# New orders in the opening of a linear-attention and expert kernel: lanes in three buffers, another bank for the first w, half of X loaded from ScalarE's queue

## The chip, the cores and the metric

The kernel runs on one core of one Trainium2 chip. The metric is the device time in microseconds (us), the median of the runs. The core has TensorE (PE), VectorE (DVE), ScalarE (ACT), GpSimd (POOL) and SyncE (SP), whose queue here only issues DMAs. Each engine works through its own instructions in the order written and waits on semaphores.

## What is computed

A recurrent attention over 768 tokens for 4 batches of 8 heads of size 40, then a gated expert layer and a second one over the 3072 x 320 result:

```python
for t in range(S):
    y[:, :, t] = np.einsum('bhd,bhde->bhe', rt, state)
    Sa = np.einsum('bhde,bhe->bhd', state, at)
    state_decay = state * wt[:, :, None, :] - np.einsum('bhd,bhe->bhde', Sa, bt)
    state = state_decay + np.einsum('bhd,bhe->bhde', vt, kt)
...
h = (x @ w1) * (x @ w2) @ w3
x = h @ w_out
out = np.maximum(x @ w_in, 0.0) ** 2 @ w_out2
```

## The kernel before

The recurrence is cut into 24 windows (n): 64 tokens of two of the four batches, all heads in pairs side by side. Even and odd windows are the two halves of the batches, so window n takes its state from window n - 2. For each window TensorE turns w, a and r (ar), b and k (bk) with transposes (`turn_w`, `turn_ar`, `turn_bk`); VectorE forms the running product of w (`scan`), its reciprocal (`invert_decay`, two parts), and scales a and bk by them (`scale_a`, `scale_bk`). `cross` multiplies them to 64 x 64 blocks in PSUM; `mask_ak` on VectorE copies the odd half's 32-row diagonal blocks to `diag` and masks the products; `copy_blocks` on ScalarE copies the even half's blocks to `diag` and the off-diagonal ones to `n10`. `fill_lanes` on VectorE transposes `diag` into the tile `blk` (two slots, n % 2), and GpSimd's `invert` solves the triangular blocks with 62 dependent small operations after a seed copy: windows 0 and 1 each alone, 2 and 3 in one joint pass, and each later one alone. It waits first for `inverse_turned` (the earlier inverse has left `inv`), then for `lanes_filled`. `turn_inverse` on VectorE turns the result to `invT`. Then comes the window's dependent chain: `make_z`, `make_u0`, `make_x1`, `add_x1`, `make_u1`, `turn_uv`, `add_state`, `new_state`, `make_read`, `mask_read`, `make_y`, `turn_state`, `scale_y`, with copies out of PSUM on ScalarE between them (`copy_x`, `copy_u`, `copy_uvT`, `copy_state`). Windows 0 and 2 use the PSUM tensor `both` and 1 and 3 `aside`; from 4 on all use `both`, since the experts take `aside`.

y goes to DRAM (`store_y`, tensor xT) and comes back as X (`load_x`, x_raw), is split into a rounded and a rest part (`round_x` on ScalarE, `rest_x` on VectorE) and multiplied with split weights. The products of w3 and w_out are folded once in the opening: `turn_w3(ft)` and four `multiply_w3(ft, part)` for each of 8 row blocks, then `round_fold`, `rest_of_fold`, `store_fold`. The weights come by `load_staged`, w_out as `load_wo`.

The opening is the first four windows and the fold; its order is written out by hand, one list for each engine. After it a loop over windows 4 to 23 weaves the window's steps with steps of the expert layers (`next(beside)`), and after window 23 only experts are left. The first expert matmul (xT_hi, `into_hidden`) stands in that loop after the whole opening list of TensorE. The lists wait across engines: on SyncE `next_w(n)`, `next_ar(n)` and `next_bk(n)` wait for the transposes of window n - 1, since each raw tile has one buffer; `load_x` waits until the stores of y have landed; `store_fold(ft)` waits for `rest_of_fold(ft)`.

## Time and profile before

| | us |
|---|---|
| median of 3 runs (lowest, highest) | 1009.25 (1007.94, 1013.59) |
| the profiled execution | 1012.14 |
| its span | 1010.4 |
| busy in the span: PE, DVE, POOL, ACT | 953.6, 653.9, 448.4, 424.6 |
| first expert matmul | 138.49 |

The profile is one execution. Busy time is the time in which an engine's instructions run; matmuls are pipelined and their ends modelled. A line of a timeline gives start, duration, engine, line of the kernel, operation, output and input tiles, the count of merged instructions, and in brackets the idle time of the engine in front and what ended it. PEclk is the granted TensorE clock as a share of 2.4 GHz. DMA share is the mean busy share of the 16 DMA engines.

### The profile page before, as it was taken

The page shows a single profiled execution, that of the slowest core. Times are in us where ns is not written, and L with a number is a line of the kernel's source. Part 1 is how long each engine was busy: PE and PEld are TensorE (multiplying, and loading weights), DVE is VectorE, ACT ScalarE, POOL GpSimd, SP SyncE. Part 2 cuts the span into 40 slices and gives each one's busy share as a digit, 9 for nine tenths or more (in the row PEclk, how much of TensorE's full clock was granted, in tenths as well). Part 3 has the DMA queues.
Part 4 walks back from the last instruction along what each step waited for, and adds up shares of the span by engine and source line. Part 5 has one row for each costly group of instructions (what it writes and reads, how often), then busy time and mean ns, then how long its engine had stood idle before and what let it go on. Part 6 is the DMA issues. An engine that isn't in the chain of part 4 may idle for free.

```text
span 1010.4 us, 34808 instructions
## 1 busy us (share of the span) xinstructions
PE 953.6 (94%) x14560; PEld 775.6 (77%) x14560; DVE 653.9 (65%) x1101; ACT 424.6 (42%) x904; POOL 448.4 (44%) x1464
## 2 busy tenths in 40 slices
PE   5877898989898999999999999999999999999998
PEld 4665666778787778887778887778887778888797
DVE  7877556788866567667577677577677575442433
ACT  3443444455544344444345444344344344432332
POOL 2778725537446265365355355355356355100000
PEclk8999789999989999999999999999999999999999
DMA  9965466757868757658756759765758743565552
GB/s 178 180 148 124 106 153 182 187 164 229 235 203 235 148 145 168 160 145 229 168 143 161 176 140 228 158 149 154 178 146 221 158 130 123 178 205 180 156 159 78
DMA packets 267804, 169.52 MB, mean 168 GB/s; under 512 B 200064, under 2 KB 229760, under 8 KB 267648
## 3 DMA queue, kind: packets, MB, share of 16 engines
q1 hardware_dynamic: 267648, 167.29, 64.8%
q8 instruction: 116, 1.90, 0.8%
q14 instruction: 40, 0.33, 0.1%
HBM read 141.03 MB, written 26.21 MB: 166 GB/s over the span
## 4 chain that ended last, share of the span: by engine, by line
PE 69%; DVE 4%; POOL 2%; issue 2%; ACT 1%; DVEq 0%
PE aside L908 29%; PE moe_bank L995 16%; PE moe_bank L980 8%; PE both L871 2%; PE both L763 2%; PE both L886 2%; PE both L804 1%; PE both L795 1%; PE both L857 1%; PE both L776 1%; POOL inv L703 1%; PE both L882 1%; POOL inv_tmp L700 1%; PE both L743 1%; DVE h_lo L1588 1%
## 5 line engine op out<-in xcount | busy, mean ns | idle before, releaser
L700 POOL TENSOR_TENSOR inv_tmp<-blk,inv 128x60 f32<-128x60 f32 (+26 forms) x713 | 205.7, 288 | 356.2 <-DVE blk L1511 302.0
L703 POOL TENSOR_TENSOR inv<-inv,inv_tmp 128x60 f32<-128x60 f32 (+26 forms) x713 | 230.9, 324 | 55.8
L995 PE MATMUL moe_bank<-v_ring,h_hi 128*128 128x320 f32 x768 | 177.1, 318 | 0.0
L908 PE MATMUL aside<-xT_hi,w_ring 128*128 128x512 f32 x480 | 150.3, 411 | 3.5 <-DVE h_lo L1588 3.5
L908 PE MATMUL aside<-x2T_hi,w_ring 128*128 128x512 f32 x480 | 148.5, 407 | 4.0 <-DVE h_lo L1588 3.9
L995 PEld LDWEIGHTS moe_bank<-v_ring,h_hi 128*128 128x128 f32 x768 | 128.7, 189 | 6.1
L1588 DVE TENSOR_TENSOR h_lo<-aside,h_hi 128x512 fp32r<-128x512 f32 x144 | 97.4, 676 | 49.2 <-ACT h_hi L1290 49.1
L1598 DVE SCALAR_TENSOR_TENSOR aside<-aside,left 128x512 f32<-128x512 f32 x96 | 66.7, 695 | 95.3 <-ACT left L1298 95.1
L1290 ACT CAST h_hi<-aside 128x512 fp32r<-128x512 f32 x144 | 84.6, 588 | 95.6 <-DVE aside L1598 52.5
L995 PE MATMUL moe_bank<-v_ring,h_lo 128*128 128x320 f32 x384 | 119.2, 310 | 0.0
L1298 ACT ACTIVATE left<-aside 128x512 f32<-128x512 f32 x96 | 57.5, 598 | 115.9 <-PE aside L908 115.7
L908 PEld LDWEIGHTS aside<-xT_hi,w_ring 128*128 128x128 f32 x480 | 85.4, 189 | 22.0 <-DVE h_lo L1588 5.0
L908 PEld LDWEIGHTS aside<-x2T_hi,w_ring 128*128 128x128 f32 x480 | 84.1, 188 | 22.0 <-issue 5.4
L908 PE MATMUL aside<-xT_lo,w_ring 128*128 128x512 f32 x288 | 98.2, 395 | 0.0
L908 PE MATMUL aside<-x2T_lo,w_ring 128*128 128x512 f32 x288 | 97.0, 391 | 0.0
L1475 DVE RECIPROCAL undecay<-decay 104x256 f32<-104x256 f32 x48 | 83.4, 1740 | 0.2
L980 PE MATMUL moe_bank<-h_hi,v_ring 128*128 128x512 f32 x240 | 81.6, 405 | 0.0
L1236 ACT COPY uv<-both 32x160 f32<-32x160 f32 x176 | 49.8, 283 | 61.4 <-PE both L804 59.8
L995 PEld LDWEIGHTS moe_bank<-v_ring,h_lo 128*128 128x128 f32 x384 | 72.7, 189 | 0.0
L1596 DVE TENSOR_TENSOR aside<-left,aside 128x512 f32<-128x512 f32 x48 | 33.0, 687 | 55.0 <-PE aside L908 54.7
L908 PEld LDWEIGHTS aside<-xT_lo,w_ring 128*128 128x128 f32 x288 | 54.9, 191 | 12.5
L908 PEld LDWEIGHTS aside<-x2T_lo,w_ring 128*128 128x128 f32 x288 | 54.1, 188 | 12.5 <-DVE x2T_lo L1630 0.2
...
## 6 DMA issues: line engine op xcount, KB each, us to landing
...
```

The costliest lines, as they stand in the source:

```text
L700: nc.gpsimd.tensor_tensor(tmp, x[:, :, j, 0:j].unsqueeze(3).broadcast_to(shape), mine[:, :, j:j + 1, lo:X].broadcast_to(shape), ALU.mult). ...
L703: nc.gpsimd.tensor_tensor(mine[:, :, 0:j, lo:X], mine[:, :, 0:j, lo:X], tmp, ALU.add).then_inc(solve, 1)
L908: last = nc.tensor.matmul(bank(use), w, x, start=n == 0, stop=n == len(terms) - 1)
L980: last = nc.tensor.matmul(bank(f"x{m}"), weights[:, lo:lo + P], h[at % RING][:], start=f == 0 and n == 0, stop=f == FT - 1 and n == len(te ...
L995: last = nc.tensor.matmul(bank(f"o{s}")[:, 0:M], h[at % RING][:, s * P:(s + 1) * P], weights[:, rest * M:(rest + 1) * M], start=f == 0 and ...
L1236: last = nc.scalar.copy(uv[n % 2][rows, odd::2, q, 0:D], solved(n, q, at, odd))
L1290: nc.scalar.copy(h_hi[at % RING][:], hidden_at(x)).then_inc(hi_made, 1)
L1298: nc.scalar.activation(left[x % 2][:], hidden_at(x), ACT.Relu).then_inc(taken, 1)
L1475: nc.vector.reciprocal(undecay[0:E, xs], decay[n % 4][0:E, xs, 1:C + 1]).then_inc(undecayed, 1)
L1588: nc.vector.tensor_tensor(h_lo[at % RING][:], hidden_at(x), h_hi[at % RING][:].bitcast(F32), ALU.subtract).then_inc(lo_made, 1)
L1596: nc.vector.tensor_tensor(into, left[x % 2][:], into, ALU.mult).then_inc(combined, 1)
L1598: nc.vector.scalar_tensor_tensor(out=into, in0=into, scalar=0.0, in1=left[x % 2][:], op0=ALU.max, op1=ALU.mult).then_inc(combined, 1)
```

## The change

- `blk` has three slots. Window 0 uses slot 2, windows 1, 2 and 3 use 0, 1 and 2; later windows use n % 2. The copies to `diag` are steps of their own (`gather_low` on ScalarE, `gather_high` on VectorE) with semaphores of their own; `fill_lanes` waits for these two, not for a mask, and for window 3 for the inversion of window 0. ScalarE's second copy to `n10` waits for `gather_high` instead of the first mask.
- The first w is turned into the second half of `aside`; the ar transposes of window 0 no longer wait for the scan, and turn_w(1) does.
- The opening lists of SyncE, TensorE, ScalarE and VectorE are in a new order. `load_x(0, 0)` is issued from ScalarE's queue, after `copy_state(3)`; `load_x(0, 1)` stays on SyncE's.

The diff, with indentation cut and parts of the lists left out:

```diff
-blk = sb("blk", [P, 2, BLK, BLK])
+blk = sb("blk", [P, 3, BLK, BLK])
...
-solve = sem("solve")
+solve, low_gathered, high_gathered = sem("solve"), sem("low_gathered"), sem("high_gathered")
...
+def its_w(n):
+
+    return its_second(n if n else 1)
...
+def lane_slot(n):
+    return (2, 0, 1, 2)[n] if n < OPENING else n % 2
...
     begin(inputs.w_loads(0))
     begin(inputs.ar_loads(0))
     begin(inputs.bk_loads(0))
+    next_w(1)
+    next_ar(1)
     load_staged(0)
-    next_w(1)
+    next_bk(1)
     sp.wait_ge(cleared, len(clears))
+    next_w(2)
     begin(inputs.zv_loads(0))
-    next_ar(1)
     load_wo()
-    next_bk(1)
+    next_ar(2)
+    begin(inputs.zv_loads(1))
     load_staged(1)
-    begin(inputs.zv_loads(1))
-    next_w(2)
+    next_bk(2)
+    next_w(3)
     begin(inputs.uv_loads(0))
     load_staged(2)
-    next_ar(2)
+    next_ar(3)
     begin(inputs.uv_loads(1))
+    store_fold(0)
     next_staged(3)
+    next_bk(3)
+    next_w(4)
+    next_staged(4)
     next_zv(2)
-    next_bk(2)
-    next_staged(4)
-    store_fold(0)
-    next_w(3)
...
+    store_fold(6)
+    load_v(0)
+    load_v(1)
     store_y(2)
-    load_x(0, 0)
     store_y(3)
     load_x(0, 1)
+    next_uv(4)
+    store_fold(7)
     next_staged(11)
-    load_v(0)
-    load_v(1)
-    store_fold(6)
-    store_fold(7)
+    next_uv(5)
     load_v(2)
     load_v(3)
...
-        halves = slice(n % 2, n % 2 + count)
-        x, mine = blk[:, halves], inv[:, halves]
+        at_lane = lane_slot(n)
+        x, mine = blk[:, at_lane:at_lane + count], inv[:, n % 2:n % 2 + count]
         wait(pool, inverse_turned, n + count - 2)
         nc.gpsimd.tensor_copy(mine, inv_unit[:].unsqueeze(1).broadcast_to([P, count, BLK, X])).then_inc(solve, 1)
         pool.wait_ge(lanes_filled, n + count)
...
         pe.wait_ge(loaded_w, 32 * (n + 1))
         if n <= OPENING:
             wait(pe, rows_copied, n - 1)
+            if n == 1:
+                pe.wait_ge(decayed, 1)
...
-            last = nc.tensor.transpose(its_second(n)[0:E, x * P:(x + 1) * P], pair(w_raw, x), ident[:])
+            last = nc.tensor.transpose(its_w(n)[0:E, x * P:(x + 1) * P], pair(w_raw, x), ident[:])
...
         pe.wait_ge(loaded_ar, 32 * (n + 1))
-        pe.wait_ge(decayed, n + 1)
+        if n:
+            pe.wait_ge(decayed, n + 1)
...
     turn_w(0)
     turn_ar(0)
     turn_bk(0)
+    turn_w(1)
+    cross(0)
+    turn_ar(1)
     turn_w3(0)
-    cross(0)
-    turn_w(1)
+    turn_bk(1)
+    multiply_w3(0, 0)
     turn_rows(0)
+    turn_w(2)
+    cross(1)
     make_z(0)
-    turn_ar(1)
-    multiply_w3(0, 0)
     multiply_w3(0, 1)
+    turn_ar(2)
     multiply_w3(0, 2)
-    turn_bk(1)
+    turn_w3(1)
     multiply_w3(0, 3)
-    turn_w3(1)
-    cross(1)
-    turn_w(2)
     multiply_w3(1, 0)
+    turn_bk(2)
+    multiply_w3(1, 1)
+    turn_w3(2)
     turn_rows(1)
-    multiply_w3(1, 1)
+    cross(2)
     make_z(1)
-    turn_ar(2)
+    turn_w(3)
     multiply_w3(1, 2)
-    turn_w3(2)
+    multiply_w3(2, 0)
     multiply_w3(1, 3)
-    turn_bk(2)
-    multiply_w3(2, 0)
+    turn_ar(3)
+    multiply_w3(2, 1)
     turn_w3(3)
-    cross(2)
-    turn_w(3)
-    multiply_w3(2, 1)
+    make_u0(0)
+    turn_bk(3)
+    multiply_w3(2, 2)
+    make_x1(0)
+    multiply_w3(2, 3)
+    turn_w3(4)
+    make_u1(0)
+    cross(3)
+    turn_uv(0)
     multiply_w3(3, 0)
-    make_u0(0)
-    turn_ar(3)
-    make_x1(0)
-    multiply_w3(2, 2)
+    add_state(0)
     multiply_w3(3, 1)
-    turn_bk(3)
-    make_u1(0)
-    multiply_w3(2, 3)
-    turn_uv(0)
+    multiply_w3(4, 0)
+    make_read(0)
     multiply_w3(3, 2)
-    cross(3)
-    add_state(0)
-    multiply_w3(3, 3)
-    turn_w3(4)
-    make_read(0)
-    multiply_w3(4, 0)
-    turn_w3(5)
+    multiply_w3(4, 1)
     make_y(0)
     turn_state(0)
...
+    turn_w3(7)
     make_u0(2)
+    multiply_w3(6, 1)
     make_u0(3)
     make_x1(2)
+    multiply_w3(6, 2)
     make_x1(3)
     make_u1(2)
     make_u1(3)
     turn_uv(2)
     turn_uv(3)
     add_state(2)
-    multiply_w3(5, 3)
+    multiply_w3(6, 3)
     make_read(2)
-    multiply_w3(6, 0)
+    multiply_w3(7, 0)
     add_state(3)
     make_y(2)
     turn_state(2)
     make_read(3)
-    turn_rows(4)
+    multiply_w3(7, 1)
     make_y(3)
     turn_state(3)
+    turn_rows(4)
+    multiply_w3(7, 2)
     make_z(4)
     turn_ar(5)
-    multiply_w3(6, 1)
-    turn_w3(7)
-    multiply_w3(6, 2)
+    multiply_w3(7, 3)
     turn_bk(5)
-    multiply_w3(6, 3)
-    multiply_w3(7, 0)
     cross(5)
-    multiply_w3(7, 1)
-    multiply_w3(7, 2)
-    multiply_w3(7, 3)
...
+    def load_x(i, h):
+        tile = xT_dram.rearrange("k (b s) -> k b s", b=B)[:, 2 * h:2 * h + 2, 2 * C * i:2 * C * (i + 1)]
+        wait(act, x_split, 3 * i)
+        act.wait_ge(y_stored[h], 64 * 2 * (i + 1))
+
...
+            nc.scalar.dma_start(into(slice(lo, lo + REM), 2), tile[2 * P:M]).then_inc(x_loaded, 16)
...
-    def copy_blocks(n):
+    def gather_low(n):
         act.wait_ge(crossed, n + 1)
         wait(act, lanes_filled, n)
         for at in range(2):
             rows = slice(BLK * at, BLK * (at + 1))
-            nc.scalar.copy(diag[rows], of_half(n, 0, rows)[:, :, BLK * at:BLK * (at + 1)])
+            last = nc.scalar.copy(diag[rows], of_half(n, 0, rows)[:, :, BLK * at:BLK * (at + 1)])
+        last.then_inc(low_gathered, 1)
+
+    def copy_blocks(n):
+        act.wait_ge(crossed, n + 1)
         for q in range(2):
             lo = DP * q
-            wait(act, masked_ak, (2 * n + 1) * q)
+            if q:
+                act.wait_ge(high_gathered, n + 1)
             nc.scalar.copy(n10[n % 4][lo:lo + BLK], of_half(n, q, slice(lo, lo + BLK))[:, :, BLK:C]).then_inc(
                 blocks_copied, 1)
...
     copy_r(0)
+    gather_low(0)
+    copy_r(1)
+    copy_blocks(0)
     copy_w3(0)
-    copy_blocks(0)
     copy_rows(0)
...
     copy_uvT(3)
     place_state(3)
     copy_state(2)
+    copy_state(3)
+    load_x(0, 0)
     copy_rows(4)
-    copy_state(3)
     copy_x(4)
     copy_r(5)
-    copy_w3(7)
-    round_fold(6)
+    round_fold(7)
     round_x(0)
-    round_fold(7)
...
         if one:
+            gather_low(n + 1)
             copy_blocks(n + 1)
...
         dve.wait_ge(turned_w, n + 1)
-        w_turned = its_second(n)[0:E].rearrange("e (x b t) -> e b x t", x=X // 2, b=2)
+        wait(dve, y_scaled, n - 3)
+        w_turned = its_w(n)[0:E].rearrange("e (x b t) -> e b x t", x=X // 2, b=2)
...
+    def gather_high(n):
+
+        dve.wait_ge(crossed, n + 1)
+        wait(dve, lanes_filled, n)
+        for at in range(2):
+            rows = slice(DP + BLK * at, DP + BLK * (at + 1))
+            last = nc.vector.tensor_copy(diag[rows], of_half(n, 1, rows)[:, :, BLK * at:BLK * (at + 1)])
+        last.then_inc(high_gathered, 1)
+
     def mask_ak(n):
         dve.wait_ge(crossed, n + 1)
-        for at in range(2):
-            rows = slice(DP + BLK * at, DP + BLK * (at + 1))
-            nc.vector.tensor_copy(diag[rows], of_half(n, 1, rows)[:, :, BLK * at:BLK * (at + 1)])
         for q in range(2):
             rows = half_rows(1 - q)
             nc.vector.tensor_tensor(azk[n % 2][rows, :, q, :], of_half(n, q, rows),
...
                                     ALU.mult).then_inc(masked_ak, 1)
     def fill_lanes(n):
-        dve.wait_ge(blocks_copied, 2 * n + 1)
-        dve.wait_ge(masked_ak, 2 * n + 1)
-        if n >= 2:
-            dve.wait_ge(solve, inverted(n - 2))
-        nc.vector.transpose(blk[:, n % 2], diag[:].rearrange("i x j -> i j x").unsqueeze(2).broadcast_to(
+        dve.wait_ge(low_gathered, n + 1)
+        dve.wait_ge(high_gathered, n + 1)
+        if n > 2:
+            dve.wait_ge(solve, inverted(n - 3 if n < 6 else n - 2))
+        nc.vector.transpose(blk[:, lane_slot(n)], diag[:].rearrange("i x j -> i j x").unsqueeze(2).broadcast_to(
             [P, BLK, 4, X])).then_inc(lanes_filled, 1)
...
     scale_a(0)
     invert_decay(0, 1)
     scale_bk(0)
-    mask_ak(0)
     scan(1)
+    gather_high(0)
     fill_lanes(0)
     invert_decay(1, 0)
     scale_a(1)
     invert_decay(1, 1)
+    mask_ak(0)
     scale_bk(1)
-    rest_of_fold(0)
-    mask_ak(1)
     scan(2)
+    gather_high(1)
     fill_lanes(1)
     invert_decay(2, 0)
     scale_a(2)
     invert_decay(2, 1)
-    rest_of_fold(1)
+    mask_ak(1)
     scale_bk(2)
+    rest_of_fold(0)
+    gather_high(2)
+    fill_lanes(2)
+    scan(3)
+    mask_ak(2)
     turn_inverse(0)
-    mask_ak(2)
-    scan(3)
-    fill_lanes(2)
     scale_a(3)
-    add_x1(0)
     invert_decay(3, 0)
     invert_decay(3, 1)
+    add_x1(0)
     scale_bk(3)
+    rest_of_fold(1)
     rest_of_fold(2)
+    gather_high(3)
+    fill_lanes(3)
+    new_state(0)
     mask_ak(3)
-    new_state(0)
+    mask_read(0)
+    scale_y(0)
+    turn_inverse(1)
     rest_of_fold(3)
-    mask_read(0)
-    turn_inverse(1)
-    fill_lanes(3)
-    scale_y(0)
...
+    scale_bk(4)
     mask_read(1)
-    scale_bk(4)
+    gather_high(4)
+    fill_lanes(4)
+    mask_ak(4)
     scale_y(1)
...
+    rest_of_fold(5)
+    rest_of_split(1)
     turn_inverse(2)
     turn_inverse(3)
-    fill_lanes(4)
     add_x1(2)
     add_x1(3)
-    invert_decay(5, 1)
     new_state(2)
-    rest_of_split(1)
-    rest_of_fold(5)
     mask_read(2)
+    rest_of_fold(6)
     new_state(3)
     scale_y(2)
     mask_read(3)
     scale_y(3)
     scale_a(5)
+    rest_of_fold(7)
     scale_bk(5)
+    rest_x(0)
     turn_inverse(OPENING)
-    rest_of_fold(6)
```

## Rows read from the trace of the kernel before

**Rows 1.** Busy time of each engine by stretch.

```profile
core 0: us, PE busy (x) PEld busy (x) DVE busy (x) ACT busy (x) POOL busy (x), PEclk, DMA share, GB/s
0.00:138.50 138.50, 107.59 (x2369) 81.89 (x2369) 95.05 (x172) 54.80 (x126) 86.65 (x268) 0.89 0.70 144
400.00:500.00 100.00, 99.60 (x1683) 82.01 (x1682) 68.53 (x110) 40.98 (x90) 46.52 (x158) 1.00 0.71 176
```

**Rows 2.** TensorE's timeline from 100 us: start, us, tile, idle before.

```profile
start us, us, engine line op out<-in xcount [idle before <-releaser]
100.95 0.76 PE L804 MATMUL both<-x_row,invT 32*32 32x40 f32 x32 [4.02 <-DVE invT L1517]
...
110.94 2.31 PE L960 MATMUL moe_bank<-wo_raw,hidden 128*128 128x320 f32 x4
...
138.49 1.32 PE L908 MATMUL aside<-xT_hi,w_ring 128*128 128x512 f32 x4
```

**Rows 3.** GpSimd's timeline: seed copies, first and last products.

```profile
21.03 0.25 POOL L700 TENSOR_TENSOR inv_tmp<-blk,inv 128x31 f32<-128x31 f32 x1 [16.01 <-DVE blk L1511]
...
44.40 0.25 POOL L700 TENSOR_TENSOR inv_tmp<-blk,inv 128x31 f32<-128x31 f32 x1
...
68.29 0.61 POOL L693 COPY inv<-inv_unit 128x512 f32<-128x512 f32 x1 [0.77 <-DVE invT L1517]
70.10 0.30 POOL L700 TENSOR_TENSOR inv_tmp<-blk,inv 128x62 f32<-128x62 f32 x1 [1.19 <-DVE blk L1511]
...
99.98 0.22 POOL L703 TENSOR_TENSOR inv<-inv,inv_tmp 128x16 f32<-128x16 f32 x1
```

**Rows 4.** VectorE's timeline: window 0's blocks and lanes, and the last y_out.

```profile
15.33 0.86 DVE L1499 COPY diag<-both 32x256 f32<-32x256 f32 x2 [1.28 <-PE both L763]
...
19.01 1.94 DVE L1511 STREAM_TRANSPOSE blk<-diag 128x1024 f32<-128x1024 f32 x1
...
124.22 0.86 DVE L1561 TENSOR_TENSOR y_out<-aside,decay 40x256 f32<-40x256 f32 x2 [0.19 <-ACT st L1256]
```

**Rows 5.** The SyncE queue's issues of wo and of the last bk part.

```profile
12.16 1.53 SPq L417 DMA_DIRECT2D wo_raw<-in_moe_w_out  x2
...
16.34 1.70 SPq L388 DMA_DIRECT2D bk_raw<-in_k  x1
```

**Rows 6.** From issue to landing: the second w, then wo.

```profile
DMA to landing us min/median/max: 4.5/4.6/4.7
...
DMA to landing us min/median/max: 5.6/6.6/7.7
```

**Rows 7.** TensorE's timeline from 8 to 68 us.

```profile
8.03 1.09 PE L743 MATMUL both<-ident,ar_raw 64*104 64x64 f32 x16 [1.82 <-DVE decay L1467]
11.03 1.10 PE L753 MATMUL both<-ident,bk_raw 64*104 64x64 f32 x16 [1.91 <-DVE azk L1483]
...
27.30 1.34 PE L960 MATMUL moe_bank<-wo_raw,hidden 128*128 128x320 f32 x4
28.48 1.04 PE L948 MATMUL moe_bank<-ident,stage 128*128 128x128 f32 x8
29.45 1.16 PE L763 MATMUL aside<-azk,bkT 40*64 40x64 f32 x64
...
47.25 0.49 PE L804 MATMUL both<-x_row,invT 32*32 32x40 f32 x32
...
66.61 0.52 PE L895 MATMUL both<-ident,sT 40*40 40x40 f32 x32
```

**Rows 8.** Two stretches with the granted clock (PEclk), columns as in rows 1.

```profile
17.50:24.00 6.50, 5.45 (x91) 4.54 (x92) 6.44 (x14) 1.71 (x3) 2.34 (x9) 0.50 1.09 226
101.00:112.00 11.00, 8.64 (x258) 7.28 (x259) 7.43 (x13) 6.38 (x18) 7.28 (x25) 0.50 0.31 71
```

**Rows 9.** The SyncE queue's first issues for X and window 3's y.

```profile
127.08 0.89 SPq L410 DMA_DIRECT2D x_raw<-xT  x2
...
129.30 2.25 SPq L397 DMA_DIRECT2D xT<-y_out  x4
132.79 0.90 SPq L410 DMA_DIRECT2D x_raw<-xT  x2
```

**Rows 10.** ScalarE's timeline: the first rounding of X.

```profile
136.66 1.66 ACT L1305 CAST xT_hi<-x_raw 128x512 fp32r<-128x512 f32 x3 [2.90 <-DMA x_raw<-xT]
```

109 lines of the change are left out of this document (58 added, 51 removed).

## The prediction

> **What bounds the kernel now.** I read the busy time by stretch first [rows 1]. From 400 to 500 us TensorE is busy for 99.6 of 100 us at the full clock, and the other engines have room. An edit that touches only the opening can therefore pay in one way: the first expert matmul, at 138.49 us [rows 2], comes earlier, and all behind it moves with it. In the opening itself TensorE is busy 107.59 of 138.5 us [rows 1]; the other 31 us are gaps. So I looked for what ends last there.
>
> It is GpSimd, which inverts the 32-row blocks of window 0, of window 1, and then of windows 2 and 3 together. Its timeline [rows 3] shows them nearly end to end: the first product of window 0 at 21.03 us, of window 1 at 44.40, of the joint inversion at 70.10, and its last sum at 99.98, done at 100.20: 30.1 us. The idle time in front of each first product is put down to VectorE, which fills the lanes (tile blk) or turns the inverse (invT). After 100.2 us one dependent chain follows, u0, x1, u1, state, read and y of windows 2 and 3, which ends with the last y_out at 125.08 us [rows 4]. Then y is stored, X loaded and rounded, and the first expert matmul runs. The opening is thus: start of the joint inversion, + 30.1, + 24.9, + a tail of 13.4 us (125.08 to 138.49). I price the change in these terms. The profiled execution has a span of 1010.4 us and a time of 1012.14; the median of the runs shown is 1009.25, and I apply the shift to the median.
>
> **The change, part by part.**
>
> *Window 0's lanes.* Before, VectorE idles 1.28 us until the crossed product is there, copies its half, then masks and scans window 1 (2.8 us between the end of the copy at 16.2 and the fill at 19.01), and the fill ends at 20.95 [rows 4]. After, the scan (1.5 us) runs in the idle time and over it by 0.3 us, and the mask comes behind the fill: 20.95 - 2.8 + 0.3 = 18.4. This needs window 1's w, issued right behind bk at about 6.7 us; w landed 4.5 to 4.7 us after issue [rows 6], so by 12.1, and its transposes fit behind those of bk, done at 12.13 [rows 7]. GpSimd starts at 18.5, not 21.03: 2.5 us earlier. The other bank for the first w spares the ar transposes the 1.82 us wait for the scan [rows 7]. Their readers wait on VectorE, which has only the 1.28 us gap up to there, so I price it at nothing; were VectorE's queue no cover, it would be worth up to 1.3 us.
>
> *Window 1* follows without a hole, from about 41.8 to 65 us instead of 44.40 to 67.5 (the row of the joint seed copy at 68.29 has 0.77 us of idle time in front [rows 3]). Its lanes come at about 35 us.
>
> *The joint inversion.* Its seed copy ran at 68.29 and its first product only at 70.10, because the fill stood behind the turning of inverse 1. Filled ahead, that costs the copy alone: 1.1 us less. But it still waits for the turning of inverse 1, and in VectorE's new order scale_y(0), the last step of window 0's chain, stands in front of that. This is where the change adds a wait; behind it on GpSimd are all 30.1 us. So the question is when window 0's chain ends. Before: u0 at 47.25, turned state at 67.13 [rows 7], 19.9 us.
>
> *What window 0 waits for.* SyncE's new order has next_bk(1) ahead of zv, wo and w2, and next_bk(1) waits for the bk transposes of window 0 (12.1 us). Before, wo was issued at 12.16 [rows 5]. Now bk1 (four issues of 0.64 to 1.70 us [rows 5]; I take 3.0 in all), w2 and zv0 (1.3 each) come first: wo goes at about 17.9 and lands up to 7.7 us later [rows 6], at 25.6 (bounds 23.5 and 27). TensorE's new order has multiply_w3(0, 0), which needs wo, ahead of turn_rows(0), turn_w(2) and cross(1). Behind the bk1 transposes (done at 22.6, set by scale_a(1) on VectorE) TensorE stands until 25.6. It will then be at the low level: before, the granted clock was 0.50 (1.2 of 2.4 GHz) for all of 17.5 to 24 us, after gaps of 1.8 us [rows 7, 8]. At that level a multiply part takes 2.31 us [rows 2] and not 1.34 [rows 7]. With part 2.3, rows 1.6, ACT's copy of them 0.7, w 1.0 and cross 1.2, cross(1) ends at 32.4, not 30.61 [rows 7]. From there to u0(0) the new order has 20 items. By the start-to-start times of before at full clock (1.18 for each of nine multiply parts, 0.97 for each of three turned w3 tiles, cross 1.09 [rows 7], and 4.5 us for the other seven steps) they add up to 19.1. With 0.2 of waiting for bkT of window 2, u0(0) is at 51.7, not 47.25: 4.4 us late. VectorE leads to nearly the same: its turning of inverse 0 now stands behind copies, fill, scan and mask of windows 2 and 3, and is done at 50.8, though GpSimd finished at 41.4. From u0(0) to the turned state the new TensorE order holds 17.7 us of steps, plus 0.5 of waits: 69.9. Then scale_y(0) 1.3, turning 0.7 and the copy 0.7: the first joint product is at 72.6. The 2.5 us won in front are lost, and 2.5 more: **+2.5 us**. Bounds: with wo at 23.5 and the full clock cross(1) ends at 29.5, hence -0.4; with TensorE at half clock on to 40 us, +5.
>
> *The chain of 24.9 us.* VectorE loses a fill and a split, ACT a split, none of them on the chain. The new order puts two multiply parts between its short steps. At full clock they fit beside ACT's copies; at the low level, 2.31 us each [rows 2], they would put u1(2) back by 2.3. The clock was 0.50 over 101 to 112 us [rows 8], after a gap of 4.02 us in front of u0(2) [rows 2]. After the change 3.6 us more work (two parts and a w3 tile) stand ahead of u0(2), so the gap is about 2.5 us, and the fillers keep TensorE at work behind it: I expect a shorter low stretch and take **-0.8**, between -2.7 (all of these steps at their fast durations) and +2.3.
>
> *The tail.* Before, SyncE waited until 127.08 us to issue load_x(0, 0), and only then, at 129.30, the store of window 3's y, ready at 125.08 [rows 4, 9]. After, ACT's queue waits and issues, and the store goes at 125.2. By the same 3.5 us (129.30 to 132.79 [rows 9]) and 3.87 us (132.79 to the first rounding at 136.66 [rows 10]) X is there 7.4 us after the last y_out instead of 11.6: -4.2. But ACT now stands at load_x until y of window 2 has landed (0.4 us after the last y_out), needs 2.2 us to issue four loads (SyncE's time for them, 127.08 to 129.3), and behind it are copy_rows(4), copy_x(4), copy_r(5) and a fold. Counted from the last y_out: z(4) at 3.3 us, ar(5) at 4.8, scale_a(5) to 6.9, bk(5) to 7.6, scale_bk(5) to 8.9, cross(5) to 10.1, and the first expert matmul stands behind cross(5). So the tail is 10.1 us, not 9.2: **-3.3**, bounds -4.6 and -1. The price of a DMA issue on ACT has no row; I take SyncE's, since few transfers run beside it.
>
> Here a rule of the Trainium skill bears, in "DMA: Bandwidth & Descriptors", section "Issuing engines are not separate DMA queues": a second engine's DMAs run on the same 16 DMA engines, so it saves only the time of issuing. By it the move would be worth 2.2 us and not 3.3. No row of before can test it.
>
> *Other edits.* The w3, split and fold steps are the same instructions in new places; TensorE's gaps hide them. ACT's second n copy no longer waits for the mask, but TensorE waits for that mask itself, so nothing. Window 4's inversion starts some 1.2 us sooner for its place, and nobody waits for it before 133 us.
>
> **Sum.** +2.5 - 0.8 - 3.3 = -1.6 us: 1009.25 becomes 1007.6.
>
> **The rivals.**
>
> *A: window 0's chain is not late.* wo lands near 23.5 and the clock stays up: -0.4 - 2.7 - 4.6 = -7.7, or 1001.5. For it: a walk of twenty steps errs by a few us. Against: SyncE can't pass next_bk(1) before 12.1.
>
> *B: the joint inversion late, slower than before.* TensorE, starved at multiply_w3(0, 0), stays at 1.2 GHz, window 0's chain slides by 7 us, and scale_y(0) holds the turning of inverse 1: +5 + 2.3 - 1 = +6.3, or 1015.5. It decides from the point where that turning ends after 74.5 us. For it: the new 3 us gap. Against: TensorE has work in front of it once wo is there.
>
> *C: the experts absorb it.* The first expert matmul comes early, but the first tile then waits for split weights, whose loads (staged 10 and 11) now stand behind stores of folds and y: 1009.3. Against: the loads are not issued later than before by more than 2 us.
>
> *D: the second queue saves its issue time alone.* X's way is as long as before but for 2.2 us of issue (127.08 to 129.3 [rows 9]): +2.5 - 0.8 - 2.2 = -0.5, or 1008.7. This is what the skill's rule above would give.
>
> **How the numbers follow.** Chances: the forecast 0.37, A 0.33, B 0.15, C 0.10, D 0.05. A measurement of this kernel can tell about 0.5%, 5 us, from no change. Faster is A (0.33), slower is B (0.15), the same are the forecast, C and D (0.52). The range for 8 in 10 runs from 1000.5, a little past A, to 1013.5, and leaves out most of B and the edge of A; the likeliest case alone spans 1004 to 1012.
>
> **What would show it.** Right: GpSimd's first product near 18.5 us; a TensorE gap ending when wo lands, before turn_rows(0); u0 of window 0 near 51.7; the first joint product near 72.6, behind invT, itself right behind y_out; the store of window 3's y within 0.5 us of its scale; the first xT_hi matmul near 137. The prediction is wrong if the first joint product comes before 70 (then A) or after 74.5 (B), or if the tail from the last y_out to the first expert matmul is not 9 to 12 us.

## The result, and the profile after

The changed kernel takes 1015.72 us (median of 20 runs, 1008.87 to 1021.83), the kernel before 1009.36 (20 runs, 1003.73 to 1014.47). The ratio is 1.0064, 95% interval [1.0045, 1.0083]: slower by 6.4 us, where 1.6 us less were forecast. Single runs scatter by 2.0 to 2.7 us (standard deviation) for the kernel before and 3.5 and 4.7 us for the changed one. The profiled execution of the changed kernel took 1021.13 us, at the upper end of its runs. A second profile of the same program, taken later beside other kernels (the control below, 1014.37 us), lies near the median and stands in the last column.

The steps by which the prediction walked, in both profiles:

| us | before | predicted | after | after, control |
|---|---|---|---|---|
| GpSimd's first product | 21.03 | 18.5 | 18.80 | 18.98 |
| cross(1) ends | 30.61 | 32.4 | 32.74 | 32.54 |
| u0(0) | 47.25 | 51.7 | 52.51 | 53.72 |
| first joint product | 70.10 | 72.6 | 73.81 | 75.01 |
| joint inversion done | 100.20 | 102.7 | 103.75 | 104.97 |
| u0(2) | 100.95 | 103.4 | 109.83 | 111.35 |
| last y_out done | 125.08 | 126.8 | 134.44 | 135.30 |
| first expert matmul on X | 138.49 | 136.9 | 146.18 | 144.65 |

The last column is of the same program as the one before it. (Predicted from 72.6 on: + 30.1 to the end of the inversion; + 0.75 to u0(2) as before; + 24.1 from the inversion to the last y_out; + 10.1.) Up to the end of the joint inversion the walk holds within 1.2 us (2.4 us in the control). Then 6.08 us lie between two lines, the end of the inversion and u0(2), that stand 0.75 us apart in the kernel before; in the control it is 6.38 us. GpSimd's timeline of the changed kernel (start, duration, engine, line, operation, tiles, and the idle time in front with what ended it), against [rows 3]:

```profile
18.80 0.25 POOL L706 TENSOR_TENSOR inv_tmp<-blk,inv 128x31 f32<-128x31 f32 x1 [13.79 <-DVE blk L1552]
73.05 0.61 POOL L699 COPY inv<-inv_unit 128x512 f32<-128x512 f32 x1 [7.86 <-DVE invT L1558]
73.81 0.31 POOL L706 TENSOR_TENSOR inv_tmp<-blk,inv 128x62 f32<-128x62 f32 x1
103.53 0.22 POOL L709 TENSOR_TENSOR inv<-inv,inv_tmp 128x16 f32<-128x16 f32 x1
109.42 0.40 POOL L699 COPY inv<-inv_unit 128x256 f32<-128x256 f32 x1 [5.67 <-DVE invT L1558]
```

GpSimd is done at 103.75 and waits 5.67 us for VectorE to turn the inverse. VectorE, ScalarE and TensorE of the same kernel just ahead of u0(2), and SyncE's issues of stage 9:

```profile
107.12 0.49 DVE L1608 TENSOR_TENSOR h_lo<-moe_bank,h_hi 128x320 fp32r<-128x320 f32 x1 [2.13 <-ACT h_hi L1299]
107.52 0.68 DVE L1621 TENSOR_TENSOR w_ring<-stage,w_ring 128x512 fp32r<-128x512 f32 x1
108.22 0.42 DVE L1623 TENSOR_TENSOR w_ring<-stage,w_ring 64x256 fp32r<-64x256 f32 x1
108.67 1.22 DVE L1558 STREAM_TRANSPOSE invT<-inv 128x256 f32<-128x256 f32 x2
```

```profile
105.60 0.83 ACT L1309 CAST w_ring<-stage 128x768 fp32r<-128x768 f32 x1 [3.78 <-DMA stage<-in_moe_w]
```

```profile
107.72 1.31 PE L969 MATMUL moe_bank<-wo_raw,left 128*128 128x320 f32 x4 [2.82 <-DVE h_lo L1608]
109.83 0.49 PE L813 MATMUL both<-x_row,invT 32*32 32x40 f32 x32
```

```profile
95.29 1.51 SPq L439 DMA_DIRECT2D stage<-in_moe_w  x1
96.84 0.61 SPq L442 DMA_DIRECT2D stage<-in_moe_w  x1
97.50 0.76 SPq L439 DMA_DIRECT2D stage<-in_moe_w  x1
98.30 0.52 SPq L442 DMA_DIRECT2D stage<-in_moe_w  x1
```

Read from the bottom: SyncE issues stage 9 (split weights) from 95.29 us; in the kernel before it did so at 76.17. ScalarE stands 3.78 us at round_split(1), which needs that stage and now comes ahead of round_fold(5) and copy_w3(6). VectorE does the rests of both (107.12 to 108.64) and only then the turning, and TensorE waits 2.82 us for a freed bank before multiply_w3(6, 0), which is now ahead of make_u0(2).

The clock, too. Busy time by stretch, changed kernel (columns: stretch, length, busy time and instructions of PE, PEld, DVE, ACT, POOL, then PEclk, DMA share, GB/s):

```profile
24.00:30.00 6.00, 4.13 (x14) 2.94 (x15) 2.10 (x3) 0.69 (x1) 4.83 (x16) 0.50 1.35 196
30.00:36.00 6.00, 6.00 (x151) 4.72 (x150) 4.62 (x12) 1.77 (x5) 4.80 (x16) 0.61 0.61 103
80.00:86.00 6.00, 5.65 (x79) 4.89 (x78) 4.54 (x11) 2.63 (x8) 5.07 (x12) 0.50 0.60 169
86.00:94.00 8.00, 7.79 (x185) 6.06 (x182) 4.94 (x6) 2.33 (x5) 6.88 (x15) 0.58 0.55 95
138.00:146.00 8.00, 6.05 (x131) 4.32 (x127) 4.06 (x6) 3.10 (x6) 0.00 (x0) 0.63 0.43 112
```

The kernel before had 0.99, 1.00, 1.00 and 1.00 in the first four of these stretches: its low stretches lay at 17.5 to 24 and at 101 to 112 us [rows 8], and at 72 to 80 us, where it read 0.58 and the changed kernel 0.94. So the low stretches moved more than they grew. They do not make the gap in front of u0(2) either: in the control TensorE began the part behind which it waits, multiply_w3(5, 3), 1.9 us earlier (100.78 against 102.68), then waited 4.25 us instead of 2.82 for the rest of fold 5, and u0(2) came later still.

### The profile page after: what moved, and what is told of

Read it like the earlier page. It is cut to its first block, busy times and chain, and to the rows that moved or that the text cites. A ratio compares the mean times of both kernels' runs of the same rounds, so it can differ in the third digit from the quotient of the medians.

```text
span 1019.4 us, 34852 instructions
## 1 busy us (share of the span) xinstructions
PE 959.5 (94%) x14560; PEld 779.6 (76%) x14560; DVE 654.3 (64%) x1101; ACT 423.7 (42%) x904; POOL 445.6 (44%) x1464
## 4 chain that ended last, share of the span: by engine, by line
PE 68%; DVE 4%; POOL 2%; issue 2%; ACT 1%; DVEq 0%
PE aside L917 29%; PE moe_bank L1004 16%; PE moe_bank L989 8%; PE both L880 2%; PE both L895 2%; PE both L772 2%; PE both L813 1%; PE both L804 1%; PE both L785 1%; PE both L866 1%; POOL inv L709 1%; PE both L891 1%; POOL inv_tmp L706 1%; PE both L752 1%; DVE h_lo L1629 1%
```

## Experiments: undo one part at a time

Four theories, each tried by undoing one part of the change in the changed kernel. All ratios are to the kernel before, beside which each ran. A place in a trace is one execution; two profiles of one program differ by 1.5 us at u0(2) in the table above, so smaller differences between single traces show nothing.

**Stage 9 early** (theory: ScalarE's wait at round_split(1) holds u0(2)).

```diff
 next_zv(4)
+next_staged(9)
 next_w(5)
...
-next_staged(9)
```

> The changed kernel with one SyncE step moved: the load of the split weights 9 goes out two steps after the store of window 0's y, ahead of the wait for the state of window 1, where the changed kernel issues it at 95.3 us and ScalarE then stands 3.8 us for it (until 105.6), with copy_x(3), round_fold(5) and both w3 copies behind it. Theory (the load is late, and TensorE's own backlog stands behind it): ScalarE's wait is gone, u0 of window 2 comes about 2.2 us sooner (107.6 and not 109.8), because two multiply parts and a w3 tile still stand ahead of it on TensorE; some 2 us below the changed kernel. Rival (GpSimd alone is the bound, its result of windows 2 and 3 lay ready from 103.8 us): 4.9 us. Rival (the wait is covered): no change.

1010.93 us, ratio 1.0016 [0.9991, 1.0040]. ScalarE no longer waits, and GpSimd's next copy follows its own end again:

```profile
98.83 0.83 ACT L1309 CAST w_ring<-stage 128x768 fp32r<-128x768 f32 x1
```

```profile
74.20 0.61 POOL L699 COPY inv<-inv_unit 128x512 f32<-128x512 f32 x1 [9.32 <-DVE invT L1558]
106.23 0.40 POOL L699 COPY inv<-inv_unit 128x256 f32<-128x256 f32 x1 [0.76 <-DVE invT L1558]
```

So this wait was real and worth 4 to 5 us (1.0016 against 1.0064 and, in the control, 1.0058): the gap of 5.67 is 0.76, though the joint inversion itself began 1.15 us later than in the changed kernel. From the end of the joint inversion to the last y_out it took 23.1 us, where the kernel before took 24.9 and the changed kernel 30.7.

**wo early** (theory: the wait for wo starts the delay of window 0). In the diffs steps that stand on lines of their own in the lists are put on one where there are several.

```diff
+load_wo()
 next_bk(1)
...
-load_wo()
```

> The changed kernel with w_out's load issued ahead of next_bk(1), at about 10.6 us instead of 17.9. Theory (my prediction's step: TensorE starved at multiply_w3(0, 0) and then at 1.2 GHz until 35 us): the 2.0 us gap before 25.0 is gone, cross(1) ends about 2 us sooner, the full clock is back earlier, u0 of window 0 comes at 49 to 50 us instead of 52.5 and the joint inversion at 71 instead of 73.7; some 3 us below the changed kernel. Rival (that gap is covered by VectorE): u0 of window 0 within 1 us of 52.5 and no change in time.

1011.12 us, ratio 1.0001 [0.9979, 1.0023]. u0(0) comes at 49.33 us instead of 52.51 and the joint seed copy at 69.53 instead of 73.05. ScalarE then waits longer for stage 9, 4.62 us instead of 3.78: part of the gain turns into that wait. u0(2) is still 3.15 us earlier than in the changed kernel (106.68). The time went back as far as with stage 9 early, although stage 9 is still late here: the two gains are not to be added, and either alone undoes most of the loss.

**Inverse 1 turned early** (theory: GpSimd isn't what ends last here, so no change).

```diff
+turn_inverse(1)
 mask_read(0)
 scale_y(0)
...
-turn_inverse(1)
```

> The changed kernel with turn_inverse(1) ahead of mask_read(0) on VectorE, so that GpSimd no longer waits 7.9 us (65.2 to 73.05) for scale_y(0). Theory (after the change TensorE and the load of split weights 9 are the bound, not GpSimd): the joint inversion starts near 67 and ends near 97 us, but u0 of window 2 stays within 1 us of 109.8, and the time does not move by more than 1 us. Rival (my prediction's model, in which the joint inversion sets the opening): some 5 to 6 us below the changed kernel.

1013.18 us, ratio 1.0022 [0.9995, 1.0050]. The interval overlaps those of the changed kernel, but the ratio lies 0.0036 and 0.0042 below its two, so a gain of some us is not excluded and the expectation of at most 1 us is not shown. In the trace, of an execution that took 1018.78 us, GpSimd starts the joint inversion 4.92 us earlier and loses it in front of its next copy, and ScalarE's wait for stage 9 grows to 5.86:

```profile
68.13 0.61 POOL L699 COPY inv<-inv_unit 128x512 f32<-128x512 f32 x1 [3.61 <-DVE invT L1558]
109.28 0.40 POOL L699 COPY inv<-inv_unit 128x256 f32<-128x256 f32 x1 [10.31 <-DVE invT L1558]
```

In this trace the prediction's main term, the joint inversion's start, did not set u0(2): with 4.92 us won there it came no earlier (111.69; 109.83 and 111.35 in the changed kernel). The kernel with all four undoings, below, shows the same.

**First X by SyncE** (theory: the tail is made by ScalarE's issues and half clock, not by X).

```diff
 # SyncE
 store_y(2)
+load_x(0, 0)
 store_y(3)
...
 # ScalarE
 copy_state(3)
-load_x(0, 0)
```

> The changed kernel with the first half of X loaded by SyncE's queue again, between the stores of y of windows 2 and 3. Theory (ScalarE stands 2.4 us issuing the four loads, 134.08 to 136.41, and copy_rows(4), z(4), ar(5) and cross(5) on TensorE follow that): copy_rows(4) about 2.4 us sooner, the last y_out to the first expert matmul 9.5 us instead of 11.7, some 2 us below the changed kernel. Rival (the store of window 3's y then waits again, as before the change): 1.7 us above it, tail 13.4 us.

1013.76 us, ratio 1.0034 [1.0014, 1.0054]; the tail is 9.8 us instead of 11.7. But the control, with ScalarE's loads in place, has a tail of 9.35 us, so the shorter tail is not shown to come from this edit: the 11.7 holds a stretch at the low clock that the control lacks. On ScalarE of the changed kernel the loads stand in front of copy_rows(4), for which z(4) waits 2.43 us on TensorE:

```profile
134.08 0.91 ACTq L1223 DMA_DIRECT2D x_raw<-xT  x2
135.03 1.38 ACTq L1225 DMA_DIRECT2D x_raw<-xT  x2
136.45 0.69 ACT L1252 COPY bk_row<-both 128x640 f32<-128x640 f32 x1 [2.59 <-issue]
```

With the loads on SyncE that copy runs at 133.66, right behind the last y, and X is rounded from 143.34, 9.0 us behind the last y_out; with ScalarE's queue it was 143.23, 8.8 us behind. In the other traces too the ways look alike: 7.8 to 9.1 us in the five with one half of X loaded from ScalarE's queue, 7.4 to 9.0 us in the four with the same order of stores and loads on SyncE. The second queue brought X no sooner and took 2.3 us of ScalarE. By the Trainium skill, "DMA: Bandwidth & Descriptors", section "Issuing engines are not separate DMA queues", DMAs that another engine issues run on the same 16 DMA engines and save only the time of issuing; the trace agrees, as far as X came no sooner.

**The changed kernel again**, as a control.

> The changed kernel once more, unchanged, as the control beside the next kernels. Each of the four single undoings came out at 1.000 to 1.003 of the kernel before, where the changed kernel had 1.0064. If the slowness is that of the kernel and not of the chip on which it ran, it is 1.005 to 1.008 of the kernel before (1015 to 1018 us); if the chip made it look slow, 1.001 to 1.003, and then the single undoings have bought less than they seemed to.

1014.24 us, ratio 1.0058 [1.0033, 1.0084]. The slowness is the kernel's. The wait for stage 9 is there again:

```profile
105.13 0.83 ACT L1309 CAST w_ring<-stage 128x768 fp32r<-128x768 f32 x1 [5.21 <-DMA stage<-in_moe_w]
```

**All four together.**

> All four undoings in one kernel: the load of stage 9 early on SyncE, wo ahead of the loads of bk1, turn_inverse(1) ahead of the mask, and the first X loaded by SyncE behind the store of window 2's y alone. My theory: each wait that goes uncovers the next one, and TensorE, which has 3.6 us more w3 work ahead of u0(2) and a stretch at half clock, is then the bound: u0(2) at about 103.4 us (before 100.95), last y_out near 128, tail 9.8, first expert matmul on X at about 137.8, and a time of about the kernel before, 0 to 2 us less. Rival, GpSimd is the bound: window 0's chain early and the lanes filled ahead put the joint inversion's start at 66, its end at 96 and u0(2) at 97; the first expert matmul then comes at about 131.5 and the time is 6 us below the kernel before.

1011.55 us, ratio 1.0025 [1.0002, 1.0049]. u0(2) at 104.81 and the tail, 8.6 us, are near my theory; the joint inversion's start at 65.81 is what the rival wanted, and it brings nothing:

```profile
65.81 0.61 POOL L700 COPY inv<-inv_unit 128x512 f32<-128x512 f32 x1 [0.76 <-DVE invT L1558]
103.83 0.40 POOL L700 COPY inv<-inv_unit 128x256 f32<-128x256 f32 x1 [7.45 <-DVE invT L1558]
```

GpSimd is done at 96.38, 3.8 us earlier than before, and idles 7.45 us; VectorE turns the inverse at 103.09, behind rests that wait for TensorE's w3 parts. The first expert matmul came at 138.21 (before 138.49), and yet the ratio stands for 2.5 us more than the kernel before. That was open.

## Experiments: the parts in the kernel before

**Fillers ahead of u0(2).**

```diff
 turn_w3(6), multiply_w3(5, 1), multiply_w3(5, 2)
+multiply_w3(5, 3), multiply_w3(6, 0), turn_w3(7)
 make_u0(2)
...
 # SyncE
+store_y(3)
 load_x(0, 0)
-store_y(3)
```

The later parts of fold 6 move up by as many places, and so does ScalarE's copy of w3 tile 7.

> The kernel before, with two of the changed kernel's ideas alone: on TensorE multiply_w3(5, 3), multiply_w3(6, 0) and turn_w3(7) moved ahead of make_u0(2), into the 4.02 us gap there (the ScalarE copy of w3 7 ahead of its copy of u), and on SyncE the store of window 3's y ahead of the load of X. My theory: the gap was idle time that costs nothing, so u0(2) stays at 101 us, and TensorE's clock doesn't fall behind it (granted clock 0.50 over 101 to 112 us before): 2.7 us from there, and 1 to 2 us from the order of store and load; first expert matmul on X at 133 to 134.5 us instead of 138.5, 1004 to 1006 us, ratio 0.995 to 0.997. Rival: the moved work ends after the inverse is there, puts u0(2) back by 1 to 2 us, and the clock falls all the same: 1009 us, ratio 1.000.

1009.08 us, ratio 1.0005 [0.9989, 1.0021]: missed. u0(2) kept its place (101.09) and the gap of 4.02 us [rows 2] was gone, but the work that was moved up left TensorE idle behind the last y (busy for 2.99 of the 6 us from 124 to 130 at a granted clock of 0.62; before 4.60 at 0.72). An idle gap that is filled with work from a later gap has only changed places.

**The lanes alone.**

> The kernel before, with the lanes alone: three buffers, filled ahead of the turning of the inverse (windows 3 and 4), all other orders as before. My theory: the fill of window 3's lanes (1.1 us behind the turning of inverse 1) leaves the path of GpSimd: first joint product at about 69.0 us instead of 70.10, end of the inversion at 98.9, u0(2) 0.7 to 1.1 us earlier, time 1 us less (ratio 0.998 to 1.000). Rival: the two further buffers and the semaphores cost nothing but bring nothing, because the turning itself waits for window 0's chain: first joint product stays within 0.3 us of 70.1, ratio 1.000.

1009.69 us, ratio 1.0005 [0.9984, 1.0025]. The trace did what was expected: the seed copy is at 68.31, the first joint product at 69.06 instead of 70.10, and u0(2) at 99.75, 1.20 us earlier. The measurement can't tell 1 us from none.

**wo late, planted in the kernel before.**

```diff
-begin(inputs.zv_loads(0))
 next_ar(1)
-load_wo()
 next_bk(1)
+next_w(2)
+begin(inputs.zv_loads(0))
+load_wo()
 load_staged(1)
 begin(inputs.zv_loads(1))
-next_w(2)
```

> The kernel before, with one of the changed kernel's orders planted: on SyncE bk of window 1, w of window 2 and zv of window 0 issued ahead of wo. wo then goes at about 18 us instead of 12.16, and TensorE's multiply_w3(0, 0) waits for it to about 25. My theory: late wo costs the changed kernel its time only through the order on VectorE, which has scale_y(0) ahead of the turning of inverse 1. Here the turning comes first, so window 0's chain slides by 2 to 4 us (u0 at 49 to 51 instead of 47.25) and GpSimd doesn't notice: joint seed copy within 0.5 us of 68.3, u0 of window 2 within 1 us of 100.95, ratio 0.999 to 1.001. Rival: TensorE's delay reaches u0 of window 2 all the same, since 3 us of its work are pushed into the gap of 4.02 us there and beyond: u0(2) at 102 to 103 and ratio 1.002 or more.

1010.44 us, ratio 1.0004 [0.9989, 1.0019]. The time went as the theory said and u0(2) came where the rival put it, but by a way that neither had: it was GpSimd that started late, not TensorE's work that filled the gap. u0(0) slips to 52.81, as late as in the changed kernel, and GpSimd does notice:

```profile
70.42 0.61 POOL L693 COPY inv<-inv_unit 128x512 f32<-128x512 f32 x1 [2.65 <-DVE invT L1517]
```

```profile
102.97 0.49 PE L804 MATMUL both<-x_row,invT 32*32 32x40 f32 x32 [2.54 <-DVE invT L1517]
138.55 1.17 PE L908 MATMUL aside<-xT_hi,w_ring 128*128 128x512 f32 x4
```

u0(2) is 2 us late and the first expert matmul is where it was (138.49): TensorE's idle time ahead of u0(2) is 2.54 us instead of 4.02, and the tail, 13.4 us before, is 11.9. The time did not show the two microseconds. Whether they are slack or the shorter tail is chance, one trace can't tell: two profiles of one program differ by as much.

**Stage 9 late, planted.**

```diff
-next_staged(9)
 next_w(5)
...
 next_zv(5)
+next_staged(9)
 next_staged(10)
```

> The kernel before, with the other suspect planted: the load of stage 9 put back on SyncE from 76.17 us to behind pass_split(0) and the loads of w and zv of windows 6 and 5, so that it is issued at about 98 to 102 us, later than in the changed kernel (95.29). My theory: the late load costs only where ScalarE's round_split(1) stands ahead of copy_w3(6). Here it stands behind copy_uvT(2), at 109.61 us, so it finds its data or waits 1 us: u0(2) within 0.5 us of 100.95, ratio 0.999 to 1.001. Rival: the load itself is what costs, by its place among the others (bk and ar of window 5, stage 10 and 11 slide): first expert matmul 2 us later or more, ratio 1.002 or more.

1010.50 us, ratio 1.0006 [0.9984, 1.0028]. Stage 9 is issued at 102.27, later than in the changed kernel, and ScalarE waits 1.09 us for it at 110.84, behind copy_uvT(2); u0(2) stays at 101.11. So the late load costs nothing that can be measured where round_split(1) stands late, and the early place of round_split(1) costs nothing like it once the load is early (the first undoing). The 5 us need both.

**Lanes, one filler and the order of store and load.**

> The kernel before, with the lanes in three buffers filled ahead, multiply_w3(5, 3) alone moved ahead of make_u0(2), and the store of window 3's y ahead of the load of X. From the trace of the lanes alone: u0(2) at 99.75 with 4.48 us of idle time in front of it, X's rounding at 134.90 with the ScalarE waiting 4.93 us for X, first expert matmul at 135.66. My theory: the moved part fits into the gap, u0(2) stays at 99.8, X is there 2 to 4 us earlier, the first expert matmul comes at 133.5 to 134.5, 4 to 5 us before that of the kernel before, and the time is 2 to 4 us less (ratio 0.996 to 0.998). Rival: the first tile takes it back, since window 4's chain (azk, u, read) sets the pace there: u0 of window 4 no earlier than 140.4 and ratio 0.999 to 1.001.

> The kernel before with the lanes in three buffers, multiply_w3(5, 3) ahead of make_u0(2) and the store of window 3's y ahead of the load of X, a second time. It had 0.9975, interval 0.9954 to 0.9995, with 12 runs. If the gain is real it is 0.996 to 0.999 again, first expert matmul near 136 us and u0 of window 4 near 140; if it was scatter of the runs, 0.9995 to 1.001 with the same places in the trace.

0.9975 [0.9954, 0.9995] the first time, 1.0007 [0.9987, 1.0026] the second, with the first expert matmul at 136.11 and 136.81. The mean of the two is 0.9991. Each interval holds for its own runs; with one alone I would have told of a gain of 2.5 us.

## Experiments: where the early inversion gets lost

**Fillers behind u0(2), on top of the four undoings.**

```diff
 # TensorE
 make_z(3)
-multiply_w3(5, 3)
 turn_w3(6)
-multiply_w3(6, 0), turn_w3(7)
 make_u0(2)
-multiply_w3(6, 1)
+multiply_w3(5, 3)
 make_u0(3), make_x1(2)
-multiply_w3(6, 2)
+multiply_w3(6, 0)
 make_x1(3)
...
 # ScalarE
-round_split(1), round_fold(5), copy_w3(7)
 copy_u(2, 0), copy_u(3, 0)
+round_split(1)
 copy_u(2, 1), copy_u(3, 1)
+round_fold(5)
...
 # VectorE
-rest_of_fold(5), rest_of_split(1)
 turn_inverse(2), turn_inverse(3), add_x1(2), add_x1(3)
+rest_of_split(1), rest_of_fold(5)
```

> The kernel with all four undoings, and besides: on TensorE multiply_w3(5, 3), multiply_w3(6, 0) and turn_w3(7) back behind make_u0(2), each later part one place back; on ScalarE round_split(1), round_fold(5) and copy_w3(7) behind the copies of u; on VectorE turn_inverse(2) and (3) ahead of the rest of fold 5 and of split 1. With the four undoings GpSimd had finished the joint inversion at 96.4 us and stood idle for 7.45 us, since VectorE turned the inverse at 103.09, behind work that waited for those TensorE parts. My theory: now GpSimd's end is what counts again: the turning at about 96.5 to 98, u0(2) at 98 to 99.5 (before 100.95), last y_out at 122.5 to 124, first expert matmul on X at 134.5 to 136 and a time 2 to 3 us below the kernel before (ratio 0.997 to 0.998). Rival: the moved parts stand in the chain's way or at the end, and the first expert matmul stays at 138: ratio 1.000 to 1.002.

1017.19 us (6 runs), ratio 1.0074 [1.0050, 1.0099]: as slow as the changed kernel or slower. The chain did come early, u0(2) at 99.82 and the last y_out done at 124.30, and then TensorE stood still for 8.33 us. TensorE and SyncE:

```profile
133.00 1.16 PE L773 MATMUL both<-azk,bkT 40*64 40x64 f32 x64 [2.17 <-DVE bkT L1525]
142.49 2.05 PE L918 MATMUL aside<-xT_hi,w_ring 128*128 128x512 f32 x4 [8.33 <-ACT xT_hi L1333]
```

```profile
110.08 0.35 SPq L447 DMA_DIRECT2D fold_rows<-h_hi  x1
127.16 1.75 SPq L404 DMA_DIRECT2D xT<-y_out  x4
132.60 0.90 SPq L417 DMA_DIRECT2D x_raw<-xT  x2
```

SyncE stood at the store of fold 5 until 110.08, since I had moved round_fold(5); eight steps queued up behind it, and window 2's y, ready at 119.3, was stored at 127.16. The same kind of fault as the one under study, made by me.

**SyncE mended.**

```diff
 next_bk(5)
-store_fold(5)
 store_y(1)
+next_w(6), next_zv(5), store_fold(5)
 next_staged(10), pass_split(1)
-next_w(6), next_zv(5)
 store_fold(6)
-load_v(0), load_v(1)
 store_y(2), load_x(0, 0), store_y(3), load_x(0, 1)
+load_v(0), load_v(1)
...
 # VectorE
+turn_inverse(OPENING)
 rest_x(0)
-turn_inverse(OPENING)
```

> The kernel with the fillers behind u0, and SyncE's order mended: w and zv of windows 6 and 5 ahead of the store of fold 5, the stores of y and loads of X ahead of the loads of folds; on VectorE the turning of inverse 4 ahead of the rest of X. My theory: there TensorE idled 8.33 us for X, which SyncE loaded at 132.60 although y of window 2 was ready at 119.3, behind ten issues that had waited for fold 5 until 110.08. Now X is loaded at 123 to 125, is there by 134, and the first expert matmul comes at 134 to 135.5 (before 138.49), u0 of window 4 at 140 to 141.5 (before 142.45); time 1 to 3 us below the kernel before, ratio 0.997 to 0.999. Rival: with GpSimd early, TensorE's work (w3 parts and chain together) is what ends at 137 to 138, or the loads of folds that are now late hold the first tile: ratio 1.000 or more.

> The kernel with SyncE mended, a second time. The first profile had the first joint seed copy at 66.03 us, u0(2) at 98.77, last y_out at 121.5, the first expert matmul at 132.98, and u0 of window 4 at 137.35, and a time of 1003.21 where the median of 12 was 1009.28. If the trace was typical and the median off by scatter: first expert matmul at 133 to 134 again and a ratio of 0.995 to 0.998. If that execution was a lucky one: the first expert matmul at 135 to 138 in this profile, with a stretch at half clock that the first profile didn't have, and a ratio of 0.999 to 1.001.

1.0002 [0.9983, 1.0021], then 0.9973 [0.9951, 0.9994]. The two profiles are of one program and differ by 3.4 us at the first expert matmul (132.98 and 136.38). TensorE at the same place, the first profile and then the second:

```profile
69.15 2.42 PE L970 MATMUL moe_bank<-wo_raw,hidden 128*128 128x320 f32 x8
```

```profile
70.91 3.87 PE L970 MATMUL moe_bank<-wo_raw,hidden 128*128 128x320 f32 x8
```

The same eight matmuls took 2.42 and 3.87 us; over 70 to 80 us the granted clock was 1.00 and 0.81. In the second profile it had fallen after a wait for VectorE of 2.38 us (0.22 in the first):

```profile
67.32 1.09 PE L892 MATMUL both<-rT,st 40*40 40x64 f32 x32 [2.38 <-DVE ruv L1587]
```

From that step to u0(1) it took 7.4 us, in the first profile 4.4: this one low stretch is 3.0 of the 3.4 us. Both profiles are of one program; why TensorE had to wait there in one and not in the other was not found. Over 229 executions of the kernels run here, an execution's span was longer by 4.8 us for each 0.01 by which its mean granted clock lay below its kernel's (correlation -0.59).

**Inverse 4 turned ahead of the rest of X, on the four undoings.** In the kernel with the four undoings the transpose stood behind it, at 139.91, ahead of window 5's block copies and mask:

```profile
139.91 0.70 DVE L1558 STREAM_TRANSPOSE invT<-inv 128x256 f32<-128x256 f32 x1
141.54 1.41 DVE L1543 TENSOR_TENSOR azk<-both,above 64x512 f32<-64x512 f32 x2
```

```profile
143.20 0.76 PE L814 MATMUL both<-x_row,invT 32*32 32x40 f32 x32 [2.65 <-DVE azk L1543]
143.89 2.08 PE L918 MATMUL aside<-xT_hi,w_ring 128*128 128x512 f32 x4
```

TensorE waited 2.65 us (before 1.72) and did the next expert matmuls at half clock (2.08 us; before 1.44). From the first expert matmul to u1(4) it took 16.9 us there and 14.8 in the kernel before, which would be most of the open 2.5 us. The changed kernel has the same order on VectorE and waited 1.75 and 1.19 us in its two profiles, so this order alone does not fix the length of the wait.

```diff
 rest_of_fold(7), scale_bk(5)
+turn_inverse(OPENING)
 rest_x(0)
-turn_inverse(OPENING)
```

> The kernel with all four undoings, and the turning of inverse 4 on VectorE ahead of the rest of X, where the kernel before has it (133.21 us) and not behind it (139.91). My theory: there the copies of the blocks and the mask of window 5 came behind it, TensorE waited 2.65 us for them at 143.20 and ran into the first tile at half clock. Now u0 of window 4 comes 0.7 us earlier (142.5), the time is 0.7 to 2 us less than with the four undoings, ratio to the kernel before 1.000 to 1.002 (it was 1.0025). Rival: this transpose cost its own 0.7 us in a place with slack, and the first tile is held by ScalarE's or SyncE's order instead: u0 of window 4 stays at 143.2 and the ratio at 1.002 to 1.003.

> The kernel with all four undoings and inverse 4 turned early, a second time. It had 0.9975, interval 0.9953 to 0.9997, first expert matmul at 136.31 and u0 of window 4 at 140.68. If that is real: 0.996 to 0.999 again. If it was scatter: 0.9995 to 1.001.

1006.88 us, 0.9975 [0.9953, 0.9997]; and again 1007.38 us, 0.9974 [0.9956, 0.9991]. The wait is 0.72 and 0.62 us, and from the first expert matmul to u1(4) it takes 13.4 and 15.2 us instead of 16.9. The gain of 5 us, from 1.0025 to 0.9975 and 0.9974, is seen twice. The traces put 1.7 to 3.5 us of it behind the first expert matmul; where the rest comes from is not shown, and part of the 1.7 to 3.5 can be low stretches.

**Both stores ahead of both loads, on SyncE mended.**

```diff
 store_y(2)
-load_x(0, 0)
 store_y(3)
+load_x(0, 0)
 load_x(0, 1)
```

> The kernel with SyncE mended, and the store of window 3's y ahead of the first load of X. There SyncE waited until 122.51 us for the landing of window 2's y and stored window 3's y only at 125.22, though it was ready at 121.5; its load went at 128.25, and TensorE idled 1.40 us for X. My theory: the store goes at 121.6, the last load at 126.5 to 127, the rounding 1.2 to 1.8 us earlier, and TensorE, which ends cross(5) at 131.6, starts the experts there without a wait: 1 us less than the kernel with SyncE mended. Rival: no change, since both loads of X go later and ScalarE rounds all of X only when both halves are there, at the same time as now.

1005.05 us, ratio 0.9941 [0.9918, 0.9965]: 5.7 us below the kernel before and the fastest of all. Both stores stand together on SyncE (from 121.97 us), the last load at 130.30 is 4.8 us behind the last y_out instead of 6.7 and 7.0, and TensorE waits 0.49 us for X instead of 1.40 and 2.42:

```profile
121.97 5.17 SPq L404 DMA_DIRECT2D xT<-y_out  x8
127.18 1.75 SPq L417 DMA_DIRECT2D x_raw<-xT  x2
130.30 1.10 SPq L417 DMA_DIRECT2D x_raw<-xT  x2
```

That is 0.9 to 1.9 us by the traces. Against the two runs of the kernel without it (mean 0.9988) the ratio fell by 0.0047; so most of that is not explained by this edit, and it ran once.

## Why the prediction was wrong

- *GpSimd's start, wo, the starved TensorE, window 0's chain.* Right: 18.80 (18.5), wo issued at 17.89 (17.9), the wait ends at 25.00 (25.6), cross(1) ends at 32.74 (32.4), u0(0) at 52.51 (51.7). The first joint product at 73.81 was 1.2 us later than said and lay 3.7 us behind the row of before: the term +2.5 should have been +3.7, and by the control (75.01) +4.9, just inside its upper bound of +5.
- *The chain of 24.9 us, "-0.8, bounds -2.7 and +2.3".* This term failed. From the end of the joint inversion to the last y_out it measured 30.7 us: +5.8, far outside its bounds (30.3 in the control, +5.4). The failed step is the sentence "VectorE loses a fill and a split, ACT a split, none of them on the chain". The split was lost behind u0(2) and put *ahead* of it: ScalarE's round_split(1) and VectorE's rest of it stood now in front of copy_w3(6) and the turning of inverses 2 and 3. And stage 9, which it needs, was never followed through SyncE's new list (issued at 76.17 before, at 95.29 after). Some 5.3 us of the 5.8 lie in front of u0(2); taking the late load away brought u0(2) to its place behind GpSimd again and the term to 23.1 us, -1.8, inside the bounds that were given for it. The prediction walked SyncE's new list for wo and not for this load. With wo early alone the time came back as far (1.0001), though stage 9 stayed late; how the two share the loss is open.
- *"3.6 us more work ahead of u0(2), so the gap is about 2.5 us."* Wrong: the gap of 4.02 was no room to spare. In the changed kernel TensorE waited 2.82 us in the midst of that work and had no gap in front of u0(2); even with all four waits mended u0(2) was at 104.81 with no gap, GpSimd having idled 7.45 us.
- *The tail, 10.1 us.* Measured 11.7, and 9.35 in the control, so the forecast stands between two profiles of one program. z(4) at 2.85 us behind the last y_out (3.3 said) and ar(5) at 4.8 (4.8) were near, and so was the price of four issues on ScalarE, 2.3 us (2.2). The 11.7 holds a multiply part at the low level (2.50 us) between ar(5) and bk(5).
- *Rivals.* B had the right size (1015.5; measured 1015.72). That is in part luck: its sum is +5, +2.3 and -1, and the profile has +3.7, +5.8 and -1.7 (the control +4.9, +5.4 and -4.1). Its reason for the first term, window 0's chain and scale_y(0) ahead of the turning of inverse 1, was right, and its deciding point, the turning of inverse 1 after 74.5, was just missed in one profile (72.99) and lies at the edge in the control, whose first joint product came at 75.01. It did not have the wait for stage 9. Of D, X's way: the rounding came 8.8 us behind the last y_out and 7.9 in the control, between the 7.4 of the forecast and the 9.4 of D, and the load on SyncE gave 9.0. A did not occur. C did not occur either, since nothing came early for it to absorb, but what was said against it was false: the loads of stage 10 began at 111.00 us and before at 101.80.
- *The form of the sum.* It added the joint inversion's start to fixed lengths. The experiments contradict that form: 4.9 us earlier on GpSimd moved u0(2) by nothing, and with all four undoings 3.8 us earlier than before left u0(2) 3.9 us later than before. The lists of TensorE, ScalarE and VectorE in front of u0(2) are a bound of their own beside GpSimd's.
